# Moving one block-sum load and its reduction in a fused attention and MLP kernel

## The reference

```python
# attention: B=2, H=8, S=768, D=64, block 32, window 16, nb = 24
k_sum = k.reshape(B, H, nb, 32, D).max(axis=3)
v_sum = v.reshape(B, H, nb, 32, D).mean(axis=3)
scores_l = where(|i - j| < 16, scale * q @ k.T, -1e9)
scores_s = scale * q @ k_sum.T + log(32)
a = softmax(concat([scores_l, scores_s]))
x = a @ concat([v, v_sum])                 # -> (B, S, 512)
h = relu(x @ w_in); conv over 3 rows; x = (h * sigmoid(conv)) @ w_out
out = x + relu(layernorm(x) @ w_ch1) @ w_ch2
```

## Time and profile before

| | |
|---|---|
| time, median of 3 runs | 482.58 us (481.8 to 483.75) |
| the profiled execution's own time | 482.58 us |
| its span | 480.9 us |
| PE busy | 466.8 us, 97% |
| DVE, ACT, POOL busy | 289.0, 211.7 and 265.3 us |
| granted clock of TensorE | 1.000 |
| DMA queue of SP | 60508 packets, 34.72 MB |

### The profile page before, as it was taken

How to read it: one execution, slowest core, us unless ns; L and a number is a source line. 1 busy time by engine, 2 the same in 40 slices (tenths; PEclk the granted TensorE clock), 3 DMA queues, 4 the chain that set the end, 5 groups by cost and what they waited for, 6 DMA issues and landing times.

```text
span 480.9 us, 7972 instructions
## 1 busy us (share of the span) xinstructions
PE 466.8 (97%) x2807; PEld 416.4 (87%) x2807; DVE 289.0 (60%) x621; ACT 211.7 (44%) x517; POOL 265.3 (55%) x409
## 2 busy tenths in 40 slices
PE   7998889999999999999999999999999999999997
PEld 7886677899998988988898889899988999899985
DVE  6998887578755795995663364267564243333333
ACT  3888788744333665634533423333401332233110
POOL 3546788999900500028788886892006378778100
PEclk9999999999999999999999999999999999999999
DMA  9997992121100200000221022112020112211003
GB/s 211 242 231 187 230 230 78 46 89 44 45 0 1 88 1 0 1 0 1 88 89 59 29 89 89 47 42 87 2 109 23 34 55 87 89 46 44 0 1 131
DMA packets 62115, 35.63 MB, mean 74 GB/s; under 512 B 48064, under 2 KB 55004, under 8 KB 61788
## 3 DMA queue, kind: packets, MB, share of 16 engines
q1 hardware_dynamic: 60508, 34.72, 26.4%
q10 hardware_dynamic: 1568, 0.39, 0.4%
HBM read 31.08 MB, written 3.15 MB: 71 GB/s over the span
## 4 chain that ended last, share of the span: by engine, by line
PE 84%; SPq 5%; DVE 4%; POOL 2%; issue 2%; ACT 1%; DMA 1%; DVEq 0%; POOLq 0%; ACTq 0%
PE two L1407 9%; PE two L1406 9%; PE two L1405 9%; PE two L1382 8%; PE two L1385 8%; PE two L1384 8%; PE two L1244 5%; PE two L1246 5%; PE two L1245 5%; PE two L1312 5%; PE two L1313 5%; PE two L1311 5%; SPq L366 2%; PE two L1195 1%; PE two L1329 1%
## 5 line engine op out<-in xcount | busy, mean ns | idle before, releaser
L1382 PE MATMUL two<-combo,wa 128*128 128x384 f32 x224 | 75.8, 338 | 0.1
L1407 PE MATMUL two<-wv,h 128*128 128x512 f32 x192 | 75.4, 393 | 0.0
L1385 PE MATMUL two<-combo,wa 128*128 128x384 f32 x224 | 75.4, 337 | 0.0
L1406 PE MATMUL two<-wv,h 128*128 128x512 f32 x192 | 75.3, 392 | 0.0
L1384 PE MATMUL two<-combo,wa 128*128 128x384 f32 x224 | 75.2, 336 | 0.0
L1405 PE MATMUL two<-wv,h 128*128 128x512 f32 x192 | 75.0, 391 | 0.0
L555 POOL TENSOR_TENSOR asum<-wst 128x256 f32<-128x256 f32 x26 | 22.7, 873 | 93.7 <-PE two L1246 50.2
L584 POOL TENSOR_TENSOR wa<-wst,wa 128x256 fp32r<-128x256 f32 x39 | 29.6, 789 | 40.9 <-ACT wa L1028 40.9
L549 POOL TENSOR_TENSOR wa<-asum,wa 128x256 fp32r<-128x256 f32 x52 | 43.8, 843 | 4.3
L518 POOL TENSOR_SCALAR pn<-ex,rinv 128x120 f32<-128x120 f32 x96 | 33.5, 368 | 21.7 <-DVE rinv L654 21.7
L1056 ACT ACTIVATE h<-u 128x384 fp32r<-128x384 f32 x32 | 16.8, 526 | 61.6 <-DVE u L858 53.8
(11 more groups left out here) (117 smaller groups left out, 1029.5 us busy)
## 6 DMA issues: line engine op xcount, KB each, us to landing
wst<-in_moe_w_ch SPq DMA_DIRECT2D x26, 512.0 KB, 3.4
vW<-in_v SPq DMA_DIRECT2D x16, 240.0 KB
kn<-in_k SPq DMA_DIRECT2D x15, 192.0 KB, 3.7
qn<-in_q SPq DMA_DIRECT2D x15, 192.0 KB, 4.0
out<-y SPq DMA_DIRECT2D x11, 256.0 KB, 2.0
vblk<-in_v SPq DMA_DIRECT2D x3, 768.0 KB, 6.7
wst<-in_moe_w_in SPq DMA_DIRECT2D x8, 256.0 KB, 3.5
wst<-in_moe_w_out SPq DMA_DIRECT2D x8, 256.0 KB, 2.8
```

The source lines that it names most:

```text
L1382: nc.tensor.matmul(o, wk[:, 0, kk], ck[:, 0, kk], start=(first and kk == 0), stop=False, skip_group_check=True)
L1385: ins = nc.tensor.matmul(o, wk[:, 1, kk], ck[:, 0, kk], start=False, stop=(kk == 1), skip_group_check=True)
L1406: nc.tensor.matmul(o, hi, vl, start=False, stop=False, skip_group_check=True)
L1407: ins = nc.tensor.matmul(o, lo, vh, start=False, stop=(f == NFP - 1 and c == 1), skip_group_check=True)
```

## The change

Two orders are changed. On DVE, the first half of the reduction for group 2, `block_sums(2, 0)`, is issued at the end of step 6, not of step 7; the second half stays in step 9. On SP, in the iteration p = 2, `load_v(3)` comes first, then `load_vsum(2)`, then `load_vblk(2)`, where `load_vsum(2)` and `load_vblk(2)` came ahead of `load_v(3)`. No instruction is added or removed.

```diff
-        SUMS = {3: ((1, 0),), 4: ((1, 1),), 7: ((2, 0),), 9: ((2, 1),), 12: ((3, 0),), 15: ((3, 1),)}
+        SUMS = {3: ((1, 0),), 4: ((1, 1),), 6: ((2, 0),), 9: ((2, 1),), 12: ((3, 0),), 15: ((3, 1),)}
@@ in the loop over p on SP @@
                 if p == 4:
                     load_vblk(3)
-                if p == 2:
-                    load_vsum(p)
-                    load_vblk(2)
                 if p + 1 < NPAIR:
                     load_v(p + 1)
-                if p != 2:
-                    load_vsum(p)
+                load_vsum(p)
+                if p == 2:
+                    load_vblk(2)
                 for n in {3: (1,), 4: (2,), 5: (3,), 7: (4,)}.get(p, ()):
                     load_w(n)
```

## The result

The changed kernel takes 486.88 us (median of 4 runs, 486.55 to 487.17), the kernel before beside it 483.16 us (481.8 to 483.75). The ratio is 1.0081, 95% interval 1.0055 to 1.0106: slower by 3.7 us. (The times given are medians. A ratio is estimated from all runs of both kernels and can differ by up to 0.15% from that of the medians.) In a second set of runs the ratio was 1.0064 (1.0039 to 1.0088), 486.33 against 483.91 us, so the loss was 2.4 us by the medians there. The forecast was 482.8, and the result lies above its range of 481.0 to 486.2.

A forecast was written before the change was run, and what follows sets the result against it. PE bounds the kernel (84% of the chain); SP's issues and the DVE loop set the attention stage to step 14. From 482.58, plus 2.9 lag, minus 2.97 covered, plus 0.2 for slipping key transposes: 482.8 us, range 481.0 to 486.2.

The forecast's parts named there:

- Issue of vblk: SP's queue, p = 2: load_vblk(2) would be issued at 33.82 instead of 30.50, 3.3 us later.
- Landing: Arrival of load_vblk(2)'s data: 5.5 us after issue, so at 39.3.
- two ends: Bounds for vblk's arrival: 3.4 us after issue (37.2) and 6.9 us after issue (40.7).
- the formula T - 36.4: DVE's lateness at score_max(9), with T the time vblk lands: 2.9 us for 39.3, 0.8 to 4.3 at the extremes.
- The cover: After step 10, a late DVE finds others ready, so its former idle times absorb 2.97 us of lateness.
- The sum of the four: DVE's later idle times before scores (0.26), vblk (0.67) and transposed keys (1.06 and 0.98), in all 2.97 us.
- Its stall: SP's 4.32 us hold at a load_v(3) transfer, ending at 37.05; it would move with vblk and end at 39.0.
- the late landing: vblk arriving 6.9 us after issue, at 40.7: lag 4.3 us, load_q(6)'s query transposes 1.4 us late.
- Rival A: DVE's queue in step 6: the 2.9 us lag is carried to the end, 485.5 us (486.9 if vblk lands late); chance 0.22.
- rows 6: Profile rows of DVE's four later idle times, 0.26, 0.67, 1.06 and 0.98 us, forecast to go.
- Rival C: PE idle from 39.8 to about 43.1 drops its clock for two steps: +1.2 us, 484.0; chance 0.06.
- Rival B: SP's issues decide: earlier vblk landing lets SP get up to 3 us ahead, about 481.4 us; chance 0.12.

The follow-up runs named there:

- SP's half alone: Changed kernel with SP's new transfer order, but block_sums(2, 0) back in step 7: 484.51 us, ratio 1.0012 against the kernel before.
- the version with its clock kept: Changed kernel plus 32 more identity transposes on PE in its idle gap of step 7: 485.36 us, ratio 1.0034 against the kernel before.
- the one extra reduction: Kernel before plus one extra 1.9 us DVE reduction into scratch in step 7: 483.79 us, ratio 1.0002; with two such reductions 485.43 us, ratio 1.0037.
- the DVE half alone: Kernel before with only block_sums(2, 0) moved to step 6, SP's order unchanged: 482.99 us against 483.94, ratio 0.998.
- with vblk early: Kernel before with block means and weights ahead of values, load_vblk(2) ahead of load_vsum(2), block_sums(2, 0) in step 6: 481.70 us, ratio 0.9970.
- the versions with the block means first: Kernel before with SP issuing block means and weights ahead of values: 480.94 us; second version, more such loads ahead of keys and queries: 480.90; both ratio 0.9942.

## Why the prediction was wrong, point by point

**Issue of vblk.** 33.82 forecast, 33.83 measured. Right.

**Landing.** I took 5.5 us between two ends; it took 6.9, the upper end, and vblk was there at 40.7. The lag by the formula T - 36.4 is then 4.3; 4.17 was measured. The formula held, its input was 1.4 us low. All three loads that I had read took 6.3 to 6.9; 5.5 lay under every one, with a reason (a sparser queue) that no row of the same load supported. In the second profile of the changed kernel the load was issued at 34.7 and took 5.6, so it landed at 40.3; SP's half alone has 34.7 and 6.5, the version with its clock kept 35.2 and 5.7. In this order of SP it landed between 40.3 and 41.2 in these four, though the issues lie 1.4 us apart. With the landing put right and nothing else, my own sum gave 484.1 at most, so this is only a part.

**"The loop around DVE is tight in steps 8 to 10, and I carry 2.9 us through them."** It grew there: from 4.17 at `score_max(9)` to 54.81 - 49.40 = 5.41 at the key transposes. The clock is the part of this that a run separates: 0.66 us by the profiles above. The other 0.6 us is not split further. It is tempting to give it to `row_sums(8)`, which takes 0.73 us instead of 0.16 beside a POOL instruction (last section). But in the second profile of the changed kernel `row_sums(8)` takes 0.16, and from `score_max(9)` to the key transposes it is 10.77 us there, against 10.85 here and 9.61 before. The chain shown above does not pass through it either: it runs from POOL at 44.12 over PE at the lower clock. In the version with its clock kept that row is long too, so the clock alone may be worth more than 0.66.

**The cover, the step that failed.** "The sum of the four is 2.97 us. Lag left over: 2.9 - 2.97, nothing." What was covered, against the profile that I had read, is 1.48 + 0.26 = 1.74 us (5.41 to 3.93 to 3.65 at the three key transposes). I had added up DVE's idle times as if a late DVE would find everybody else ready. But 0.67 and 0.48 us of its two idle times before `key_max` belong to the loop itself: PE's transposes there wait for PE's outputs, which wait for ACT's copies, POOL and DVE. They stay, whatever the transfers do: 2.97 less these two is 1.82. Only the part above the floor of 9.7 us a pair was slack. The same holds for PE's 0.76 us at 69.97, which names no releaser and which I put down to a transfer: 0.42 of it stands ahead of the key transposes in the changed kernel too (row at 63.91).

The sum with the measured terms, for the two profiled executions: 4.17 + 1.24 - 1.74 = 3.67 us, where the outputs of step 18 were 3.64 us late and the executions differ by 486.00 - 482.58 = 3.42. Against the forecast's lag of 2.9 and cover of 2.97, three terms are off, each by about 1.2 us: the landing (1.27), the growth in steps 8 to 10 (1.24) and the cover (1.23).

**SP.** Its stall moved with vblk and ended at 40.5, and `load_q(6)` waited for the query transposes until 50.1, as said for the late landing. It cost nothing: the third vblk load, 2.3 us later than before, was in place when DVE came at 60.54.

**The rivals.** Rival A, the lag carried to the end, is what happened; its 486.9 for the late landing is the measured median. It had 0.22, and its condition was the right question ("if the idle times of rows 6 are not true slack"): I had the argument for it in hand, the closed loop, and did not work out the loop's floor, which the distance between key transposes gives, 38.94 - 29.22 = 9.72 us in the kernel before. Rival C happened beside it, in all runs: 0.7 to 1.0 us, less sure than the rest, for the forecast 1.2. It was put up as something that excludes A, when the gap that A makes is what triggers it. The Trainium skill's rule ("TensorE: Matmul & The Clock Gate", "HAM oscillation — how this bites in real kernels"), that a gap in which PE waits puts its clock back, agrees with the windows above: 0.52 and 0.50 after 4.87 us of idleness. Rival B did not show.

**The base.** The profile of before came from an execution of 482.58. Later medians were 483.16, 483.94, 483.91 and 483.48. It holds less waiting for transfers than its usual run, so against the usual run more is covered than 1.74: the one extra reduction was free, and 2.3 us of two were covered. That is part of why the second set of runs shows a loss of 2.4 us and not of 3.7. Cover is no constant of the kernel; it is what the execution that one compares with had lost above the floor. I read 2.97 us from an execution that had 1.74 to give.

What stays open: why the load of vblk takes between 5.6 and 6.9 us, what the part of the growth in steps 8 to 10 is that the clock doesn't explain, and by what the DVE half alone came out 0.9 us faster although its profiled run has a longer wait.

## What to carry to other kernels

When several engines form a loop, find its floor first, as the distance of one repeated instruction in stretches without any wait for a transfer. A new lateness is covered only by what the loop runs above this floor, never by the sum of one engine's idle times, for part of each is the loop's own. Before a consumer is moved ahead, take the landing of its data and not its issue, at the upper end of what the trace shows; and look to the transfers first: here an order by due time was worth 3.0 us, and it took most of the spread between runs with it.

## What the runs showed of the hardware

A tiny DVE instruction can last as long as the POOL instruction beside it. In the changed kernel `ra` of 128x4 elements takes 0.73 us (row at 45.98 above) while POOL subtracts in the same stretch, and 0.16 us in the kernel before, where POOL is at rest:

```profile
45.97 0.73 POOL L525 TENSOR_TENSOR win<-wst,win 128x256 fp32r<-128x256 f32 x1
```

```profile
41.80 0.16 DVE L649 TENSOR_SCALAR ra<-rs 128x4 f32<-128x4 f32 x1
```

The first two end within 0.01 us of each other, and step 6 of the kernel before shows the same pair (34.11 and 34.06, 0.70 and 0.73 us). In the second profile of the changed kernel both start at 45.53, and DVE's takes 0.16 us, POOL's 0.75. The Trainium skill, "SBUF — State Buffer", section "Who interferes with whom", says that GpSimd shares a port pair with a vector instruction in a two-port mode, which a `tensor_scalar` can enter, and that whoever issues first holds it for a whole instruction while the other stands still; the durations agree. Whether a moved instruction meets such a POOL operation is a matter of phase. It is not 0.57 us on the path: POOL started its next scaling 0.34 us after its subtraction (47.03), where in the second profile it followed at once (46.26), and the way to the key transposes was as long there.

In the kernel before, the changed one and the versions with their orders on SP, SP stood still for some 3.4 to 5.3 us at the third or fourth transfer behind each load of 768 KB, and the hold ended 0 to 1.1 us before that load landed (before: 4.32 us from 32.73, 0.35 us ahead of the landing). With other transfers in between it moved: with vblk early it is 2.91 us at the fifth transfer and ends 0.5 us after the landing, and in the versions with the block means first the hold behind the third load comes at the fifth transfer or later and ends 2 us after the landing. So what ends it is not shown. What stands third or fourth behind such a load can be held for some 4 us; an order has to put what is due first ahead of it.
